# Attention unit 0: probabilities times v in plain fp32 on two 64-column groups; later splits in another order

## The reference, cut to what matters

```python
scores = scale * np.matmul(q, k.transpose(0, 1, 3, 2)) + bias     # bias: h @ w2, from log distances
attn = np.exp(scores - np.max(scores, axis=-1, keepdims=True))
attn = attn / (np.sum(attn, axis=-1, keepdims=True) + 1e-09)
x = np.matmul(attn, v)                    # heads side by side: 2304 tokens x 512
h = x @ w_in;  x = (h - np.tanh(h)) @ w_out              # 512 -> 2048 -> 512
g = x @ w_gate; val = x @ w_val                          # 512 -> 1536
out = (g * sigmoid(g) * val) @ w2_out                    # -> 512
```

## Time and profile before

| | us |
|---|---|
| median of 3 runs | 1246.85 (1246.32 to 1247.82) |
| the profiled execution, its own time | 1247.15 |
| its span, first to last instruction | 1245.3 |
| PE busy | 1178.9 (95% of the span) |
| PEld busy | 1094.1 (88%) |
| DVE busy | 625.8 (50%) |
| ACT busy | 578.8 (46%) |
| POOL busy | 531.6 (43%) |

### The profile page before, as it was taken

One profiled execution on the slowest core, in us unless ns is written; L12 is line 12 of the kernel. 1 busy time (PEld: TensorE's weight loads), 2 busy tenths in 40 slices (PEclk: granted clock), 3 DMA queues, 4 the chain that ended last, 5 costly groups with the idle time before them and its releaser, 6 DMA issues.

```text
span 1245.3 us, 20293 instructions
## 1 busy us (share of the span) xinstructions
PE 1178.9 (95%) x7312; PEld 1094.1 (88%) x7312; DVE 625.8 (50%) x1401; ACT 578.8 (46%) x1171; POOL 531.6 (43%) x600
## 2 busy tenths in 40 slices
PE   5776699999999999999999999999999999999998
PEld 2356699999999998999899999999999999999998
DVE  8978777766566656666666634421211212112111
ACT  6976667665556555555555544521212222122212
POOL 2046577765555555777777722111111111111111
PEclk9989899999999999999999999999999999999999
DMA  5886466343434333545545353300100000000000
GB/s 175 261 251 189 134 188 193 104 140 107 124 102 139 108 110 112 141 130 138 146 134 141 92 178 126 104 26 1 51 2 26 26 26 26 1 26 1 26 1 26
DMA packets 80068, 125.47 MB, mean 101 GB/s; under 512 B 19424, under 2 KB 42976, under 8 KB 79968
## 3 DMA queue, kind: packets, MB, share of 16 engines
q1 hardware_dynamic: 79968, 124.17, 34.1%
HBM read 104.07 MB, written 20.05 MB: 100 GB/s over the span
## 4 chain that ended last, share of the span: by engine, by line
PE 77%; DVE 14%; ACT 4%; issue 3%; DMA 1%; POOL 0%; DVEq 0%; SPq 0%; ACTq 0%; POOLq 0%
PE ps_y L1397 13%; PE ps_s L1489 12%; PE ps_y L1500 12%; PE ps_h L1378 9%; PE ps_h L1489 6%; PE ps_pt L1489 6%; PE ps_pt L1351 5%; PE ps_s L1318 4%; PE ps_pt L1334 4%; DVE feat L1037 4%; DVE prob L1070 3%; DVE wbuf L1086 2%; PE ps_pt L1378 1%; DVE fr L1044 1%; ACT wbuf L775 1%
## 5 line engine op out<-in xcount | busy, mean ns | idle before, releaser
L706 POOL TENSOR_TENSOR fr<-tanh_b,fr 128x384 fp32r<-128x384 f32 x72 | 72.9, 1012 | 378.2 <-ACT fr L967 378.2
L1397 PE MATMUL ps_y<-fr,wbuf 128*128 128x384 f32 x1152 | 226.0, 337 | 1.8 <-POOL fr L648 1.8
L1378 PE MATMUL ps_h<-fr,wbuf 128*128 128x384 f32 x1056 | 207.3, 340 | 4.0 <-DVE fr L1115 3.0
L643 POOL TENSOR_SCALAR prob<-prob,rowinv 128x576 f32<-128x576 f32 (+1 forms) x160 | 121.9, 762 | 206.3 <-DVE rowinv L1081 190.9
L1397 PEld LDWEIGHTS ps_y<-fr,wbuf 128*128 128x128 f32 x1152 | 198.7, 188 | 2.5 <-POOL fr L648 2.5
L1378 PEld LDWEIGHTS ps_h<-fr,wbuf 128*128 128x128 f32 x1056 | 181.5, 189 | 6.4 <-DVE fr L1115 3.1
L768 ACT ACTIVATE prob<-prob,negmax 128x576 f32<-128x576 f32 (+1 forms) x160 | 124.0, 775 | 100.0 <-DVE negmax L1070 99.4
L1500 PE MATMUL ps_y<-wbuf,fr 128*128 128x512 f32 x648 | 161.1, 393 | 0.0
L648 POOL TENSOR_TENSOR fr<-g_b,fr 128x384 fp32r<-128x384 f32 x96 | 97.3, 1013 | 104.3 <-ACT fr L792 104.3
L1500 PEld LDWEIGHTS ps_y<-wbuf,fr 128*128 128x128 f32 x648 | 120.5, 188 | 22.1
L1086 DVE TENSOR_TENSOR wbuf<-ps_pt,wbuf 128x512 fp32r<-128x512 f32 (+1 forms) x144 | 97.0, 674 | 46.1 <-ACT wbuf L775 44.3
(11 more groups left out here) (128 smaller groups left out, 1997.1 us busy)
## 6 DMA issues: line engine op xcount, KB each, us to landing
biasb<-bias_scratch SPq DMA_DIRECT2D x128, 216.0 KB, 2.8
raw<-k_t SPq DMA_DIRECT2D x59, 288.0 KB, 3.0
bias_scratch<-w_raw SPq DMA_DIRECT2D x72, 144.0 KB, 3.3
biasb<-bias_scratch SPq DMA_DIRECT2D x64, 144.0 KB, 2.9
w_raw<-w_chunks SPq DMA_DIRECT2D x16, 512.0 KB, 5.5
prob<-w_chunks SPq DMA_DIRECT2D x8, 768.0 KB, 4.7
raw<-v_p SPq DMA_DIRECT2D x32, 160.0 KB, 2.2
biasb<-bias_scratch SPq DMA_DIRECT2D x64, 72.0 KB, 2.6
```

The lines of the kernel that those rows point to most:

```text
L643: eng.tensor_scalar(row, row, rowinv[0:hd.rows, tile % PR:tile % PR + 1], 1.0, ALU.mult, ALU.mult).then_inc(p_norm, 1)
L1378: mm = eng.matmul(hidden_bank(u, c)[:, 0:TOK], w[:, cols], x[:, d, :], start=d == 0 and i == 0, stop=d == KC - 1 and i == 2)
L1397: mm = eng.matmul(ps_y[:, d, 0:TOK], w[:, cols], g[c % 2], start=c == 0 and i == 0, stop=c == C1 - 1 and i == 2)
```

## The change

For the heads of unit 0 (`plain(hd)`), the probabilities are no longer split: `pt_copy` (ACT) and, for the packed keys, `pt_copy_end` (DVE) copy them as fp32 into a double buffer (`plain_of`), laid over a raw buffer of w1 instead of over `wbuf`. v isn't split either; PE reads it from `v_raw`. `output_plain` multiplies in fp32 with 64 stationary columns: even chunks go to PSUM rows 0 to 63, odd chunks to rows 64 to 127, the packed keys to rows 0 to 63. v of head n-1 is loaded in SP's round n, after `output` of head n-2, and no longer one round earlier after `split_v`. In the `edge`, `output` moves ahead of transposes 2, `x_high(0)` and `x_low(0, 0)` to the front. At every later hand-over `x_high_last` and `x_low(u, 1)` move into the old unit's last slot, and hidden pieces wait for all of x. In slots of three-tile heads, `pt_low_end` moves ahead of the last `score` (unless the slot begins a unit), and POOL's `split_g` ahead of `norm` 1 in a slot that begins a unit. In `short` slots that begin a unit, DVE takes `pt_low` 1 and `score` 1 ahead of `inverse` 0 and `q_low`, ACT orders its copies anew, and PE does three pieces instead of two ahead of `output`.

```diff
             def load_v(hd):
-                wait(eng, p_vlo, hd.n)
+                if hd.n <= H:
+                    wait(eng, e_o, hd.n)
+                else:
+                    eng.wait_ge(p_vlo, hd.n)
                 src = v_p[hd.seq * H + hd.h, :, :].rearrange("p (c d) -> p c d", c=JC)
...
-                load_v(hd)
+                if n > 1:
+                    load_v(HEADS[n - 1])
...
+            load_v(HEADS[H - 1])
...
-                    edge = q.n == H
-                    if edge:
-                        split_v(v)
                     if p is not None:
                         split_k(p, moe)
                     for t in range(q.nt):
                         norm(q, t)
-                        if t == 0 and v is not None and not edge:
-                            split_v(v)
...
                 norm(q, 0)
-                if not begins(moe):
-                    split_g(*moe[0])
+                split_g(*moe[0])
                 norm(q, 1)
-                if begins(moe):
-                    split_g(*moe[0])
                 split_k(p, moe)
...
+            def pt_copy(hd, t):
+                eng.wait_ge(e_pt, rounds(hd, t) + 1)
+                if t == 0:
+                    wait(eng, e_o, pt_free(hd))
+                eng.activation(plain_of(hd)[:, 0:FULL, tile_cols(hd, t)], by_chunk(pt_bank(t, []), hd), ACT.Copy)\
+                   .then_inc(a_pt, 1)
...
             def alone(q, v, p, moe):
                 for t in range(q.nt):
                     if v is not None:
-                        pt_high(v, t, moe)
+                        pt_copy(v, t)
                     if t == 0 and p is not None:
                         q_high(p, moe)
                     exp_tile(q, t)
-                if v is not None:
-                    pt_high_end(v)
                 if q.n >= 2:
                     o_part(HEADS[q.n - 2], moe)
 
             def edge(q, v, p, moe):
-                for t in range(v.nt):
-                    pt_high(v, t, moe)
+                pt_copy(v, 0)
+                x_high(0)
+                for t in range(1, v.nt):
+                    pt_copy(v, t)
                 o_part(HEADS[v.n - 1], moe)
-                pt_high_end(v)
-                eng.wait_ge(e_score, q.tile0 + 1)
-                x_high(0)
                 exp_tile(q, 0)
                 o_part(v, moe)
                 q_high(p, moe)
...
@@ -867,24 +886,26 @@
                 pt_high(v, 0, moe)
                 if first:
                     y_out(u - 1, [0])
+                    pt_high(v, 1, moe)
+                    exp_tile(q, 0)
+                    q_high(p, moe)
+                    y_out(u - 1, [1, 2])
+                    exp_tile(q, 1)
+                    o_part(v, moe)
+                    tanh(u, c)
+                    g_high(u, c)
+                    y_out(u - 1, [3])
+                    return
                 if p is not None:
                     q_high(p, moe)
                 if q is not None:
                     exp_tile(q, 0)
-                if not first:
-                    tanh(u, c)
+                tanh(u, c)
                 pt_high(v, 1, moe)
-                if first:
-                    y_out(u - 1, [1])
-                else:
-                    g_high(u, c)
+                g_high(u, c)
                 o_part(v, moe)
                 if q is not None:
                     exp_tile(q, 1)
-                if first:
-                    y_out(u - 1, [2, 3])
-                    tanh(u, c)
-                    g_high(u, c)
                 if late(moe):
                     x_high(u + 1)
...
+            def pt_copy_end(hd):
+                eng.wait_ge(e_pt, all_rounds(hd))
+                wait(eng, e_o, pt_free(hd))
+                eng.tensor_copy(plain_end(hd), ps_pt[64:P, 0:TOK]).then_inc(v_pt, 1)
...
@@ -1135,27 +1161,23 @@
                     score(q, t, moe)
                     if t == 1 and p is not None:
                         q_low(p, moe)
-                    if v is not None:
-                        pt_low(v, t, moe)
                     if t > 0:
                         inverse(q, t - 1)
                 if v is not None:
-                    pt_low_end(v)
+                    pt_copy_end(v)
                 if q.n >= 2:
                     x_out(HEADS[q.n - 2], moe)
                 inverse(q, q.nt - 1)
 
             def edge(q, v, p, moe):
-                for t in range(v.nt):
-                    pt_low(v, t, moe)
+                x_low(0, 0)
                 x_out(HEADS[v.n - 1], moe)
-                pt_low_end(v)
+                pt_copy_end(v)
                 score(q, 0, moe)
-                x_low(0, 0)
-                inverse(q, 0)
                 x_out(v, moe)
                 x_high_last(0)
                 x_low(0, 1)
+                inverse(q, 0)
                 score(q, 1, moe)
                 q_low(p, moe)
                 score(q, 2, moe)
...
                 u, c = moe[0]
                 first = begins(moe)
                 pt_low(v, 0, moe)
+                if first:
+                    score(q, 0, moe)
+                    pt_low(v, 1, moe)
+                    score(q, 1, moe)
+                    inverse(q, 0)
+                    q_low(p, moe)
+                    x_out(v, moe)
+                    inverse(q, 1)
+                    gated(u, c)
+                    return
                 if q is not None:
                     score(q, 0, moe)
                 if p is not None:
                     q_low(p, moe)
                 if q is not None:
                     inverse(q, 0)
-                if not first:
-                    gated(u, c)
+                gated(u, c)
                 pt_low(v, 1, moe)
                 if q is not None:
                     score(q, 1, moe)
-                if first:
-                    x_high_last(u)
-                    x_low(u, 1)
                 x_out(v, moe)
+                if late(moe):
+                    x_high_last(u + 1)
+                    x_low(u + 1, 1)
                 if q is not None:
                     inverse(q, 1)
-                if first:
-                    gated(u, c)
                 if late(moe):
                     x_low(u + 1, 0)
 
...
                 pt_low(v, 2, moe)
                 if not first:
                     q_low(p, moe)
+                    pt_low_end(v)
                 for t in range(2, q.nt):
                     score(q, t, moe)
                 if first:
                     inverse(q, 1)
-                pt_low_end(v)
-                if first:
+                    pt_low_end(v)
                     q_low(p, moe)
...
                 if late(moe):
+                    x_high_last(u + 1)
+                    x_low(u + 1, 1)
                     x_low(u + 1, 0)
...
                 elif hd.n:
                     last = HEADS[hd.n - 1]
-                    eng.wait_ge(v_pt, rounds(last, t) + 1 if t else all_rounds(last))
+                    if t == 0:
+                        eng.wait_ge(v_pt, splits(last, 0) + 1)
+                    else:
+                        eng.wait_ge(a_pt, copies(last, t) + 1)
...
             def transposed_end(hd, moe):
-                eng.wait_ge(v_pt, rounds(hd, hd.nt if moe else 1))
+                if moe:
+                    eng.wait_ge(v_pt, splits(hd, hd.nt))
+                else:
+                    eng.wait_ge(a_pt, copies(hd, 0) + 1)
...
+            def output_plain(hd):
+
+                bank = ps_y[:, 3, 0:TOK]
+                eng.wait_ge(a_pt, copies(hd, hd.nt))
+                eng.wait_ge(d_v, V_SUM[hd.n])
+                wait(eng, v_x, hd.n)
+                for c in range(0, FULL, 2):
+                    for i in range(2):
+                        eng.matmul(bank[64 * i:64 * i + 64, :], v_raw[:, c + i, :], plain_of(hd)[:, c + i, :],
+                                   start=c == 0, stop=i == 1 and c == FULL - 2)
+                eng.wait_ge(v_pt, splits(hd, 0) + 1)
+                mm = eng.matmul(bank[0:64, :], v_raw[64:P, FULL, :], plain_end(hd), start=False, stop=True)
+                mm.then_inc(e_o, 1)
...
                         if c == 0:
-                            eng.wait_ge(v_xlo, u * 2 + 1)
-                    if d == KC - 1 and c == 0:
-                        eng.wait_ge(v_xlo, u * 2 + 2)
+                            eng.wait_ge(v_xlo, u * 2 + (2 if u else 1))
+                    if d == KC - 1 and (u, c) == (0, 0):
+                        eng.wait_ge(v_xlo, 2)
...
             def edge(q, v, moe):
-                for t in range(v.nt):
-                    transposed(v, t, moe)
-                output(HEADS[v.n - 1], moe)
+                transposed(v, 0, moe)
+                transposed(v, 1, moe)
+                output_plain(HEADS[v.n - 1])
+                transposed(v, 2, moe)
                 transposed_end(v, moe)
                 scores(q, 0, moe)
                 scores(q, 1, moe)
-                output(v, moe)
+                output_plain(v)
```

(53 more changed lines are left out.)

## The result

The changed kernel takes 1259.83 us (1257.73 to 1260.65, 4 runs), the kernel before 1246.67 us (1246.32 to 1247.82, 4 runs): a ratio of 1.0101, interval 1.0084 to 1.0119. It is 13.2 us slower (from the medians). The forecast was 1236.9 us, faster, with a range of 1229 to 1243. The profiled execution took 1260.17 us, span 1258.4.

What follows compares the result with a forecast made beforehand. PE bounds the kernel from 160 us on; in unit 0 a loop of waits does. 1247.15 - 10.1 (unit 0) - 4.9 (units 1 to 3) + 5.0 (hand-overs) = 1237.15, as median 1236.9 us; range 1229 to 1243.

Steps and rivals of the forecast that it cites:

- the part on units 1 to 3: Dense slots: early packed split ends twelve PE waits, 3.1 us; early split of g ends two, 1.8; gain 4.9 us.
- The rivals: Store not late, 1230 us (0.20); loop closes elsewhere, 1242 (0.13); column groups in turn, 1244 (0.07); low clock, 1255 (0.06).
- a low clock in unit 0: PE stays at 1.2 GHz through unit 0, slots of 9.4 us, 1255 us in all; chance 0.06.
- signs of being right: Unit 0 transposes 6.9 us apart; product 2.1; no packed-split wait after 160 us; 3 us stands entering units 4, 5, lower clock after.
- signs of being wrong: Slots above 7.5 us, PE waiting on v's load, granted clock below 0.9 in unit 0, or a store as early as before.
- The fp32 product: Unit 0's plain fp32 product with v: three turns on overlapping column groups, 2.1 us, against 1.81 before.
- the two column groups run one after the other: Unit 0's product takes 3.55 us without overlap, slots 7.6 us, 1244 us in all; chance 0.07.
- agrees on the passes: Bias network row said to fit four fp32 passes, shared by column groups: 1.21 us, not 3.84; the price didn't need it.
- Unit 0's slot: Slot set by DVE's list, sum 6.7 us, taken as 6.9 with signals, against 8.42 before; gain 1.5 per slot.
- The v loop: Unit 0: product 2.1 us, then signal and load of v 3.9, until the next product: 6.0, just inside 6.7.
- Unit 0 in all: Gain 10.1 us: 7.5 from slots of heads 3 to 7, 1.2 from head 2's, 1.4 from the edge, with rounding.
- The hand-overs and `split_g`: Entering units 4 and 5, late q_low delays the store of y: 2.5 us lost each, 5.0; early split of g gains 1.8.

## Why the prediction was wrong, step by step

**The step that failed** is in the part on units 1 to 3: "The score that moves back has a slot's rest as cover." It put the packed split ahead of the last score at a gain of 3.1 us, for the twelve waits of the earlier trace rows that go. They went. But the score's cover was not the slot's rest; it was 0.06 to 0.09 us. I followed PE, where the score's result isn't needed until the next slot's transposes of tile 2, and not the lists of ACT and DVE, in which exp, tanh, gate, `g_high`, `o_part` and `x_out` stand behind that score, and PE's next transposes behind `x_out`. Counted from the start of that score, the chain needs 3.88 + 0.70 = 4.58 us to release the transposes. PE arrived there after 4.67 before (314.05 - 309.38), because in that slot its product with v (L1351) waited for the packed split, which stood behind the score. Now that product starts 0.27 us after the score instead of 1.41, with the same work behind it, so PE arrives after 3.56 and stands 1.02 us. That is one slot of twenty; twelve of them had the wait at L1351 before, in the others PE got there as late without one. The move alone costs 17.8 us in the kernel before, 19.2 in the changed one (13.2 + 6.1), where I had -3.1. That accounts for the whole miss: 1236.9 + 3.1 + 19.2 = 1259.2, measured 1259.83. Of the 19.2, the waits hold 17.7 (25.3 us at L1362 for `x_out` against 4.4 + 3.2 with the split back). The two traces also differ in unit 0's edge, by 2.0 us (14.21 and 12.26, more on it below), which is about the rest. Reordering ACT so that the chain is cut, with the split left early, ends the twenty waits and gives 1235.78; this shows the chain as the cause, and not the split's place as such. That this is near the forecast's 1236.9 is no proof of the forecast, since it is another kernel.

The rivals didn't hold it either: their one slower case was a low clock in unit 0. The granted clock was 1.00 in the slots from 99.09 to 126.40 us, and 0.89 from 118 to 148 us in both kernels, so the 1255 us of that rival had nothing to do with the result. The signs named beforehand didn't find the step either. All four signs of being right showed, the lower clock behind one of the two stands only; of the signs of being wrong three showed too, a slot of 7.70 us, PE waiting for v and a granted clock below 0.9 in the edge. None of them looked at the slots of units 1 to 3 for a new wait.

**The fp32 product**: 2.1 us forecast, 2.25 measured, so "the two column groups run one after the other" (3.55) is out. The split of that price was right too: two pairs in 1.46 (forecast 1.42), the packed keys in 0.79 (0.71). The Trainium skill ("FP8 and Floating Point Precision", TensorE Precision Notes) gives four passes for true fp32; an estimate from that for the four matmuls of the two pairs, 16 passes of 384 columns one behind the other at 2.4 GHz, is 2.56 us, and the trace shows 1.46, so the two groups share most of that time. The prediction's "agrees on the passes" says more than its row does: 1.21 us fit four shared passes (3.84 / 4 = 0.96 us), they don't show them.

**Unit 0's slot**: 6.9 forecast, 6.83 on average. The engine named was wrong, and that the average fits is luck: three of the four slots took 6.53 to 6.54 us and one 7.70. I had DVE's list at 6.7 and PE's side at 6.2, hidden by 0.5. In the chain DVE has only score and packed copy; PE's side closes the loop in 110.41 to 112.17 (1.76), 105.63 to 107.21 (1.58), 2.25 for the product and 0.95 to the next score: 6.54. DVE's sum fell short because `q_low` took 0.56 us and not the 1.36 read beside POOL's k split, which makes it 5.9. The rows tell when it is slow. The POOL instruction beside the `q_low` of 1.36 us (121.03), timeline of the kernel before:

```profile
120.54 1.44 POOL L627 TENSOR_TENSOR fr<-raw,wbuf 128x576 fp32r<-128x576 f32 x1
```

It ran already when `q_low` began and ended at 121.98; `q_low` ended at 122.39, 0.41 later. All six long ones of unit 0 end 0.41 to 0.42 us behind a POOL instruction that was already running. In the changed kernel `q_low` began at 115.13, 0.10 ahead of POOL's L650, and took 0.56. So `q_low` is long where POOL's instruction is first, and short where it is first itself; no run changed this order alone. The v loop, forecast at 6.0, set the slot of 7.70: from a product's end at 109.46 to the next product at 114.86 are 5.4 us, where I had 3.9: SP was issuing bias loads from 109.13 to 110.37 and came to v at 110.41 only.

**Unit 0 in all**: -10.1 forecast, -10.0 measured by itself. Its parts are less near: the edge's sum, 13.6 - 12.5, is 1.1, and I had put it at 1.4. From the end of the sixth `x_out` to score 2 of head 8, windows of the kernel before, of unit 0's part alone and of the changed kernel:

```profile
135.25:148.87 13.62, 11.24 (x59) 9.91 (x57) 9.88 (x20) 6.29 (x11) 4.91 (x6) 0.87 0.31 87
```

```profile
127.25:138.89 11.64, 10.05 (x56) 6.27 (x55) 7.05 (x16) 5.35 (x10) 4.54 (x4) 1.00 0.29 83
```

```profile
127.40:141.61 14.21, 13.16 (x56) 7.94 (x55) 7.06 (x16) 5.34 (x10) 4.50 (x4) 0.76 0.23 64
```

With unit 0's part alone the slots gave 8.0 us (135.25 - 127.25) and the edge 2.0. In the changed kernel's trace the same instructions of PE took 3.1 us more, at a granted clock of 0.76, and the edge was 0.6 us longer than before; so unit 0 was 7.3 us ahead there, and not 10. Why the clock fell in one execution's edge and not in the other's stays open.

**The hand-overs and `split_g`**: +5.0 - 1.8 = +3.2 forecast; the kernel with the packed split back less the one with unit 0 alone gives +3.9 (1240.89 - 1236.99). The mechanism of the store is shown by the run that issues it first. Of its sizes, the stands are 2.67 and 2.09 us instead of 3.3, and the lower clock followed only the second. The 3.3 had PE done from 487.1 us, but the row at 486.86 ends at 487.57; by that row it would have been 2.8. The gain of `split_g`, 1.8, is not there as a sum: its two waits of 0.9 went, and two of 1.0 at L1362 for L1107 came at the same hand-overs. By the rows, DVE's two `x_low` (L1141, 259.69 to 262.32) now stand ahead of the first probability split (262.35), for which the transposes at 263.18 wait. With `o_part` ahead of `g_high` `x_out`, and so `x_low`, came earlier, and these two waits were gone.

**The sum with measured terms**: 1246.7 - 10.0 + 3.9 + 19.2 = 1259.8. It has to come out, because each term is the step from one measured kernel to the next on the way from the kernel before to the changed one. What tells is each term against its forecast: -10.0 for -10.1, +3.9 for +3.2, +19.2 for -3.1.

## What to carry to other kernels

Before an instruction is moved back in an engine's list, follow everything behind it in that list, across engines, to the next thing that the bounding engine does, and measure the slack of that chain from the rows: a chain without a wait in the trace may have 0.1 us to spare, and a move of 0.6 us then costs 1 us in every slot. A small wait on the bounding engine (0.26 us, twelve times) can be the sign that its list and the others' are already in balance; remove it only with the chain behind it counted. When a move does pay with a delay, look for what stands needlessly between the delayed work and its waiter: with the split early, `o_part` behind `g_high` cost 24 us here (13.2 + 11.2, each against its own before), and without it the early split is worth 5.1 us over the late one. The store of y behind `load_q` cost 4.5.

## What the hardware showed that I hadn't expected

The length of PE's stand did not decide the clock after it. In the changed kernel PE stood 2.67 us before the transposes at 501.76 and went on at full clock; it stood 2.09 us before those at 623.51, which took 1.03 us instead of 0.60. Windows of the changed kernel:

```profile
488.00:512.00 24.00, 20.34 (x138) 18.93 (x137) 13.58 (x33) 12.89 (x29) 13.24 (x16) 1.00 0.48 148
...
623.50:627.00 3.50, 3.49 (x15) 3.50 (x16) 2.04 (x6) 1.73 (x5) 2.19 (x4) 0.51 0.39 137
```

The 0.51 is nearly all at the lower of the two levels, 1.2 GHz, and lost 3.5 x 0.49 = 1.7 us. The forecast had drawn a line between stands of 2.14 and 3.14 us from two cases in unit 0; two cases don't make a line, and the kernel with `o_part` ahead of `g_high` shows the same: stands of 2.19 and 2.01 us, granted clock 1.00 after the first and 0.57 after the second. With the second buffer for v a stand of 2.61 us was followed by 0.65, where the changed kernel's 2.67 at the same place was followed by 1.00.
